# Gated attention and two feed-forward layers on one core: the fourth attention unit's states and output ahead of other work, the fifth unit three slots later

## What is computed

```python
def _attn_ref(q, k, v, f_logit):            # batch 4, 8 heads, 768 tokens, head size 48
    f = 1.0 / (1.0 + np.exp(-f_logit))
    for t in range(S):
        state = f[:, :, t, :, None] * state + np.einsum('bhd,bhe->bhde', k[:, :, t], v[:, :, t])
        y[:, :, t] = np.einsum('bhd,bhde->bhe', q[:, :, t], state)

def _moe_ref(x, w_a, w_b, w_out):           # x: 3072 tokens x 384; w_a, w_b: 384 x 1536
    return (x @ w_a) * (x @ w_b) @ w_out

def _moe2_ref(x, domain_probs, w1, w2):     # 4 experts of 1024
    p = domain_probs / (domain_probs.sum(-1, keepdims=True) + 1e-09)
    for e in range(E):
        out += p[:, e:e + 1] * (np.maximum(x @ w1[e], 0.0) @ w2[e])
```

## Time and profile before

| | |
|---|---|
| median of 3 runs | 1345.38 us (1344.77 to 1345.45) |
| the profiled execution | 1345.9 us, of which the span of instructions is 1344.2 us |
| PE busy | 1327.3 us, 99% of the span |
| DVE, ACT, POOL busy | 864.4, 602.0, 575.3 us |
| PE's granted clock, mean | 0.994 |

### The profile page before, as it was taken

How to read it: one execution, slowest core, us unless ns; L and a number is a source line. 1 busy time by engine, 2 the same in 40 slices (tenths; PEclk the granted TensorE clock), 3 DMA queues, 4 the chain that set the end, 5 groups by cost and what they waited for, 6 DMA issues and landing times.

```text
span 1344.2 us, 23409 instructions
## 1 busy us (share of the span) xinstructions
PE 1327.3 (99%) x8187; PEld 1300.6 (97%) x8187; DVE 864.4 (64%) x1681; ACT 602.0 (45%) x1227; POOL 575.3 (43%) x575
## 2 busy tenths in 40 slices
PE   8899999999999999999999999999999999999999
PEld 7899999999999999989999999999999999999998
DVE  8776556556543332346777687777777776777765
ACT  4544434434332222344545644545554546454541
POOL 4452212313215767124444744445644446544441
PEclk9899999999999999999999999999999999999999
DMA  6543322223203334213232234332243222342221
GB/s 166 158 114 65 66 46 67 62 50 67 54 10 97 123 113 123 79 59 95 85 94 77 85 100 129 95 93 78 84 134 94 88 80 69 119 123 92 88 65 48
DMA packets 80166, 118.77 MB, mean 88 GB/s; under 512 B 8112, under 2 KB 61872, under 8 KB 80048
## 3 DMA queue, kind: packets, MB, share of 16 engines
q1 hardware_dynamic: 80048, 117.26, 30.8%
HBM read 100.58 MB, written 14.55 MB: 86 GB/s over the span
## 4 chain that ended last, share of the span: by engine, by line
PE 95%; DVE 1%; issue 1%; ACT 1%; DMA 1%; ACTq 0%; DVEq 0%; SPq 0%
PE bank L1675 12%; PE bank L1677 11%; PE bank L1676 11%; PE bank L1875 10%; PE bank L1876 10%; PE bank L1877 10%; PE bank L1769 8%; PE bank L1771 7%; PE bank L1770 7%; PE bank L1640 2%; PE bank L1670 2%; PE bank L1663 1%; PE bank L1649 1%; PE bank L1847 1%; PE bank L1846 1%
## 5 line engine op out<-in xcount | busy, mean ns | idle before, releaser
L1148 POOL TENSOR_TENSOR wu<-w_r,wu 128x640 fp32r<-128x640 f32 (+1 forms) x132 | 200.9, 1525 | 326.1 <-ACT wu L881 326.1
L1875 PE MATMUL bank<-wd,h_hi 128*128 128x384 f32 x768 | 259.8, 338 | 0.0
L1876 PE MATMUL bank<-wd,h_hi 128*128 128x384 f32 x768 | 257.7, 335 | 0.0
L1877 PE MATMUL bank<-wd,h_lo 128*128 128x384 f32 x768 | 257.1, 335 | 0.0
L1498 DVE SCALAR_TENSOR_TENSOR xt<-bank,pn,xt 128x384 f32<-128x384 f32 x288 | 177.1, 615 | 97.0 <-PE bank L1877 87.5
L908 ACT ACTIVATE h_hi<-h 128x384 fp32r<-128x384 f32 x240 | 124.7, 524 | 196.2 <-DVE h L1448 78.3
L1769 PE MATMUL bank<-x_hi,wu 128*128 128x384 f32 x600 | 202.4, 337 | 3.6 <-DVE h L1452 2.2
L1771 PE MATMUL bank<-x_lo,wu 128*128 128x384 f32 x600 | 203.1, 339 | 0.0
L1770 PE MATMUL bank<-x_hi,wu 128*128 128x384 f32 x600 | 201.2, 335 | 0.0
L1675 PE MATMUL bank<-xs_hi,wab 128*128 128x384 f32 x576 | 196.1, 340 | 0.3 <-issue 0.3
L1676 PE MATMUL bank<-xs_hi,wab 128*128 128x384 f32 x576 | 193.2, 335 | 0.0
(11 more groups left out here) (137 smaller groups left out, 2495.9 us busy)
## 6 DMA issues: line engine op xcount, KB each, us to landing
w_r<-weight_sums SPq DMA_DIRECT2D x120, 320.0 KB, 2.9
raw<-w SPq DMA_DIRECT2D x48, 576.0 KB, 4.0
unit<-fkq SPq DMA_DIRECT2D x62, 216.0 KB, 4.1
v_in<-v_chunks SPq DMA_DIRECT2D x32, 144.0 KB, 3.9
out<-xt SPq DMA_DIRECT2D x24, 192.0 KB, 4.4
weight_sums<-w_s SPq DMA_DIRECT2D x10, 384.0 KB, 4.4
xt<-ystage SPq DMA_DIRECT2D x48, 72.0 KB, 2.2
weight_sums<-w SPq DMA_DIRECT2D x40, 64.0 KB, 2.7
```

Source lines behind the costliest of these rows:

```text
L1148: eng.tensor_tensor(wu_piece(g, n, 1), wu_raw(g, n), wu_piece(g, n, 0).bitcast(f32), ALU.subtract).then_inc(s_ulo, 1)
L1875: eng.matmul(o, hh, w_hi, start=(f == fs[0]), stop=False)
L1876: eng.matmul(o, hh, w_lo, start=False, stop=False)
L1877: mm = eng.matmul(o, hl, w_hi, start=False, stop=(f == fs[-1]))
```

## The change

```diff
-    WARM_UP, AT_TURN, AT_FFN = 35, 5, 15
+    WARM_UP, AT_TURN, AT_OUTPUT, AT_FFN = 35, 5, 4, 8
...
-    J = [APART * (u - FIRST - 1) for u in range(FIRST)] + [PACE * (u - FIRST) + 2 for u in range(FIRST, NU)]
+    J = [APART * (u - FIRST - 1) for u in range(FIRST)] + [PACE * (u - FIRST) + 5 for u in range(FIRST, NU)]
...
-    NEXT = dict(APART_FROM, limit=-7, logs=-6, sums=-5, decays=-4, gates=-4, ends=-3, keys=-2)
+    NEXT = dict(APART_FROM, limit=-8, logs=-6, sums=-6, decays=-5, gates=-5, ends=-4, keys=-4)
...
     def split_at(r):
         if r < R0:
-            return J[0] + 1 + 9 * r // 5
-        return 2 * (r - R0)
+            return J[0] + (1, 2, 4, 6, 8, 11, 14)[r]
+        return 2 * (r - R0) + (3 if PIECES_1[r][0] == 2 and PIECES_1[r][2] * OPR >= FT1 // 2 else 0)
+
+
+    def low_at(r):
+        return J[0] + 11 if r in (R0 - 3, R0 - 2) else split_at(r)
...
-        return (-3, -1, -1)[k] if n == 0 else 36 * (n - 1) + (29 if n == 1 else 20) + 2 * k
+        return k - 3 if n == 0 else 31 + k if n == 1 else 36 * (n - 1) + 20 + 2 * k
...
-                if j - 1 in SPLIT_AT and SPLIT_AT[j - 1] + 2 < R1:
-                    load_raw(SPLIT_AT[j - 1] + 2)
+                for r in range(R1 - 2):
+                    if j == low_at(r) + 1:
+                        load_raw(r + 2)
...
-                if j in SPLIT_AT and SPLIT_AT[j] < R0:
-                    first_lo(SPLIT_AT[j])
+                for r in range(R0):
+                    if j == low_at(r):
+                        first_lo(r)
...
                 if (u := at(j, "output")) is not None:
+                    if u == FIRST - 1:
+                        idle(AT_OUTPUT)
                     output(u)
```

## The result

The changed kernel takes **1346.96 us** (median of 20 runs, 1346.28 to 1349.34), the kernel before 1345.07 (20 runs, 1344.31 to 1345.89): ratio 1.0015, interval 1.0009 to 1.0022. The prediction was 1344.2, in 1341.6 to 1346.6.

The account below looks back on a forecast made before the run. PE was busy 78.00 us of 78 from 54 us, so only the head counted: first down block 2.37 earlier, less 1.14 of work moved behind it, gains 1.2; 1345.38 - 1.2 = 1344.2 us, range 1341.6 to 1346.6.

Parts of the forecast that it names:

- States, output, copies: Head: states near 32.1 instead of 34.79, output at 33.6, third unit's copy at 32.6, fourth's done by 37.3 to 38.0.
- Issue and landing of the fourth store: Head, SP: issued at 37.8 instead of 42.60, landing 4.0 later behind loads, at 42.4 against 45.4.
- Rival A: Fourth store lands early, the clock does not fall, down block near 49.4: gain 3.3, 1342.1 us; chance 0.20.
- The clock: First up block: after PE's stop from about 39.8 to 43.6 the clock is low for some 6.5 us, until 49.
- likeliest: Unit 5's limit follows the keys at once, operand at 51.35, PE starts the down block at 51.5: 1344.2 us; chance 0.47.
- Everything hangs on when the limit gets in: DVE beside POOL: limit ending at 47.15 gives the down operand at 51.35; ending at 49.0 gives 53.2.
- Rival B: Limit waits for POOL's low half of weight 7, down block at 53.2: 0.5 slower, 1345.8 us; chance 0.22.
- most cases: A DVE instruction mostly got in at the next boundary between two POOL instructions in the trace, and missed it in some.
- Equal work: Behind the head: the same work three slots later, with 1.14 us of turn and keys-values product moved behind the down block.
- DVE, ACT and POOL hide it: Steady part: the work three slots later stays hidden beside a PE that was never idle there, cost 0.

Follow-up runs that it names:

- experiment 4: Changed kernel with the load of the sixth unit's inputs issued behind the fourth unit's store: 1345.11 us, ratio 0.9999.
- experiment 3: Changed kernel with 16 filler products in PE's gap in the first up block, to keep the clock up: 1347.5 us, ratio 1.0019.
- experiment 5: Changed kernel with the splits of weight pieces 7 to 12 put in later slots: 1345.1 us, ratio 1.0003.
- experiment 14: Changed kernel with the block of weight sums and x differences put back three slots: 1346.68 us, ratio 1.0013.
- Experiments 1: Changed kernel with the fifth unit's small copy of decays put ahead of the low half of weight piece 6 on DVE: 1347.08 us, ratio 1.0015.
- 15: Kernel before with only the block of weight sums and x differences three slots later: 1346.9 us, ratio 1.0016.
- 12: Kernel before with the turn three slots later but the block of weight sums at its old slots: 1344.53 us, ratio 0.9994.
- 13: Changed kernel with sixth unit's load behind the fourth store, weight splits later, and weight sums put back three slots: 1340.68 us, ratio 0.9967.
- 8: Changed kernel with early fillers on PE near 20 us: 1347.38 us, ratio 1.0021.
- 11: Changed kernel with sixth unit's load behind the fourth store, weight splits later, and the fifth unit alone turned at its old slot: 1344.44 us, ratio 0.9994.
- 2: Changed kernel with the fifth unit's copy of decays and its limit both ahead of the low half of weight piece 6: 1346.8 us, ratio 1.0012.

## Why the prediction was wrong, step by step

- **States, output, copies: right.** States at 32.78 (near 32.1, and the masks started 0.7 late), output without a wait for `st_in`, copies at 33.83 and 37.94 (32.6 and 37.3 to 38.0).
- **Issue and landing of the fourth store: right in size, 1.3 to 1.5 late.** 39.13 against 37.8, of which 1.2 is the early delay of this profile; 4.3 to land against 4.0. X split at 43.90 against 42.4. Rival A, the early landing, did not come; experiment 4 shows what it would have taken: one load less ahead.
- **The clock: right, and harmless only behind a late gate.** Low from 43.3, as forecast; experiment 3 shows that it costs nothing in the changed kernel. With the limit in early, which is what the prediction called likeliest, PE at the low clock comes last, as the prediction had it: experiment 5 has the down block at 51.89 (forecast 51.5) and 1345.1 us, still 0.9 above 1344.2.
- **The failed step is "Everything hangs on when the limit gets in".** It took the limit to get in at the next boundary and to end 4.75 after x (47.15 against 42.4). It ended at 50.44, 6.5 after x: not because it missed a boundary itself but because `cend`, two places ahead of it, missed two. That copy was put at nothing, since it isn't in the sum at all, and it took 3.72. Without the early delay the terms stand clear: in experiment 14 x was split at 42.82, the limit ended at 49.35 and the down block started at 53.62, 2.1 behind the forecast 51.5, of which 0.4 is the landing and 1.8 the row on POOL. Rival B had the place and the price (limit after weight 7's low half, down block at 53.2), and with x 1.5 late that is the 54.7 that was measured. It had the mechanism, DVE shut out until that low half ends, but the wrong instruction, and that it fits to 0.1 is partly luck: POOL's row ended 5.6 after x and not 6.2, and the keys, which B had put in front, came behind it with their 0.56. The wrong branch was called likeliest on "most cases", which hold for single POOL instructions and for the copies beside the first of two; here three stood in a row. Experiments 1 and 5 show that this row is the cause: take the copy away and the keys pay, take the third instruction away and both are through in 2.2.
- **"Equal work": wrong in one place.** The 1.14 us of turn and keys-values product do come later, as counted. But "DVE, ACT and POOL hide it" did not hold near 545, where the weight sums moved too. The prediction named only the second block's x and the units; the table entry that depends on the last unit's slot was not followed. Alone it costs 1.6 us (15) and its removal brings 2.0 and 1.3 (12, 13), each give or take 1.2 or more; in the changed kernel 0.3 (14), which the interval cannot tell from either. The profiles show 0.12 to 1.27 of wait; whether the rest of the medians' difference is scatter or a cost that no profile caught is open.

The sum as it was, for the two profiled executions: down block 0.84 later, work moved behind it 1.14, wait near 547 0.32: 2.3, against 2.2 in the spans. Predicted for the same terms: -2.37, 1.14, 0. The 0.84 holds the early delay of 1.2. With the other profiles of either head (53.62 against 53.28 and 53.87) the first term is between -0.25 and 0.34, and with waits of 0.32 to 1.27 near 545 the sum is 1.2 to 2.8; the medians' 1.9 lies within. So of the forecast gain of 2.4 in the head next to nothing came, and the moved work and the new wait make the kernel slower.

**Open.** Why `cend` got in at the first boundary when two POOL instructions stood in a row (experiment 5: POOL's first at 44.84 for 1.28, `cend` over at 46.15) and missed it when there were three, is not shown. The number in the row doesn't decide it for other instructions: the limit at 53.69 in the kernel before stood beside three (from 53.31, 54.59 and 55.57) and got in ahead of the third, and a limit at 59.84 in the changed kernel took 2.96 beside two. That 12 is 0.8 under the kernel before may be nothing, as its interval holds 1. A lower clock of 3.4 us, after a stop of 2.2 us near 600 that all kernels have, is in some profiles (the kernel before, the changed one, 13 among them) and not in others (3, 5, 8, 11, 12); it is one source of the scatter of medians, and none of these experiments controls it.

## What to carry over

When a step is moved up so that it falls beside POOL, count how many POOL instructions stand back to back there, and price every DVE instruction beside them, the shortest too, at anything from the first boundary to the whole row: a copy of 0.15 cost 0.7 at best there and 3.72 at worst. A low clock that costs nothing behind a longer wait is to be priced anew when that wait is taken away. When a slot number moves, search for everything that is counted from it, to the end of the program, and look at each place. A store that others wait for goes ahead of loads that have time, though it is small.

## What was unexpected of the hardware

- A DVE instruction can miss the boundaries between POOL instructions: 3.72 with two of them missed (the changed kernel), 3.13 and 3.15 with one (experiments 1 and 2), against 0.98 and 1.26 where POOL had nothing behind its two products (experiment 5). The Trainium skill, "SBUF — State Buffer", section "Who interferes with whom", states of a vector instruction in a mode that uses both port pairs, a copy among others, that whoever issues first holds the shared pair for the whole instruction and the other one blocks fully. If the copy ran in such a mode, which no run shows, and came next when the first POOL instruction ended, it would have waited some 0.95 (45.80 to 46.75); the trace has 3.72, so a blocking is seen but not that end.
- The store landed later the more was queued ahead of it on SP: 4.3 behind a unit, two weights and a v, 2.6 behind two weights and a v, 2.0 to 2.2 in the quiet stretch of the earlier trace rows. The section of the Trainium skill that the prediction draws on here, "Anatomy of one DMA" in "DMA: Bandwidth & Descriptors", states its 2.0 us for transfers that GpSimd issues; these are issued by SP, and the quiet ones come nearest to it.
- At 42 to 51 us the clock at half rate for 6.8 us (experiment 3 against the changed kernel) moved the first down block by nothing (54.83 and 54.71), since PE was ahead of its operand at either rate. In experiment 5, where the operand was early, the same low clock cost about 2 us.
